# Clustered attention with two mixer layers on one core: batch 1's four one-hot pieces moved back by one tile, their buffer laid under the value copies

## The reference

```python
q_assign = np.argmax(np.einsum('bhsd,hcd->bhsc', q_n, c_n), axis=-1)
k_assign = np.argmax(np.einsum('bhsd,hcd->bhsc', k_n, c_n), axis=-1)
mask = q_assign[:, :, :, None] == k_assign[:, :, None, :]
scores = scale * np.matmul(q, k.transpose(0, 1, 3, 2))
scores = np.where(mask, scores, -1000000000.0)
...
attn = attn / (np.sum(attn, axis=-1, keepdims=True) + 1e-09)
return np.matmul(attn, v).astype(np.float32)
```

## Time and profile before

| | before |
|---|---|
| median of 3 runs | 792.05 us |
| lowest and highest of them | 791.92 and 793.27 us |
| the profiled execution's own time | 792.6 us |
| its span, first to last instruction | 790.7 us |
| mean granted clock of TensorE | 0.996 |
| PE, DVE, ACT, POOL busy | 768.8, 450.1, 361.7, 136.0 us |

### The profile page before, as it was taken

The page is one execution under the profiler, slowest core; times in us unless marked ns, Lnnn a source line. Parts: engine busy times, 40 slices in busy tenths (PEclk is TensorE's granted clock), DMA queues, the critical chain, the costliest instruction groups (busy, mean ns, idle before and its releaser), DMA issues.

```text
span 790.7 us, 12902 instructions
## 1 busy us (share of the span) xinstructions
PE 768.8 (97%) x3997; PEld 659.8 (83%) x3997; DVE 450.1 (57%) x761; ACT 361.7 (46%) x742; POOL 136.0 (17%) x162
## 2 busy tenths in 40 slices
PE   7989999999999889999999999999999999999998
PEld 6878999999999668888888888888888888888886
DVE  4778999999999684333533353334254335334333
ACT  5567888888888533323333233332123233323321
POOL 1351332233228660000300040000300000000000
PEclk9999999999999999999999999999999999999999
DMA  7935354444441223333323323333003333333334
GB/s 246 225 105 134 94 122 103 119 105 119 105 117 33 70 96 101 93 105 83 104 80 106 99 84 110 88 98 106 0 1 107 93 93 94 93 106 84 103 105 173
DMA packets 82840, 81.08 MB, mean 103 GB/s; under 512 B 7296, under 2 KB 69056, under 8 KB 82816
## 3 DMA queue, kind: packets, MB, share of 16 engines
q1 hardware_dynamic: 82816, 80.77, 37.0%
HBM read 56.95 MB, written 4.72 MB: 78 GB/s over the span
## 4 chain that ended last, share of the span: by engine, by line
PE 63%; DVE 2%; ACT 0%; issue 0%
PE bank L998 29%; PE bank L989 29%; PE bank L976 2%; PE bank L957 2%; PE bank L940 1%; DVE kT_hi L1099 1%; DVE x L1117 0%; DVE x L1150 0%; DVE w_lo L1130 0%; DVE uT_lo L1094 0%; DVE w_lo L1089 0%; DVE t L1108 0%; DVE h_lo L1126 0%; ACT qT_hi L1048 0%; ACT h_hi L1067 0%
## 5 line engine op out<-in xcount | busy, mean ns | idle before, releaser
L1126 DVE SCALAR_TENSOR_TENSOR h_lo<-bank,h_hi 128x512 fp32r<-128x512 f32 x84 | 58.1, 692 | 261.8 <-ACT h_hi L1067 261.8
L1067 ACT ACTIVATE h_hi<-bank 128x512 fp32r<-128x512 f32 x84 | 50.2, 598 | 301.4 <-PE bank L989 301.4
L989 PE MATMUL bank<-uT_hi,w_hi 128*128 128x512 f32 x336 | 131.2, 391 | 0.0
L998 PE MATMUL bank<-w_hi,h_hi 128*128 128x512 f32 x336 | 131.1, 390 | 0.0
L989 PE MATMUL bank<-uT_hi,w_lo 128*128 128x512 f32 x336 | 130.8, 389 | 0.0
L989 PE MATMUL bank<-uT_lo,w_hi 128*128 128x512 f32 x336 | 130.8, 389 | 0.0
L998 PE MATMUL bank<-w_hi,h_lo 128*128 128x512 f32 x336 | 130.7, 389 | 0.0
L998 PE MATMUL bank<-w_lo,h_hi 128*128 128x512 f32 x336 | 130.7, 389 | 0.0
L595 DVE TENSOR_TENSOR pT_lo<-back,pT_hi 128x384 fp32r<-128x384 f32 x192 | 98.1, 552 | 6.9 <-ACT pT_hi L496 3.5
L496 ACT ACTIVATE pT_hi<-back 128x384 fp32r<-128x384 f32 x192 | 84.4, 497 | 36.2 <-PE back L740 34.6
L563 DVE TENSOR_REDUCE negmax<-front 128x1 f32<-128x768 f32 x96 | 91.3, 952 | 9.2 <-PE front L639 9.2
(11 more groups left out here) (125 smaller groups left out, 1054.1 us busy)
## 6 DMA issues: line engine op xcount, KB each, us to landing
w_raw<-in_moe_w_ch_dram SPq DMA_DIRECT2D x168, 256.0 KB, 2.9
Q<-qT_hi SPq DMA_DIRECT2D x64, 96.0 KB, 2.2
K<-kT_hi SPq DMA_DIRECT2D x64, 96.0 KB, 2.1
q_raw<-in_q_dram SPq DMA_DIRECT2D x8, 384.0 KB, 6.0
k_raw<-in_k_dram SPq DMA_DIRECT2D x8, 384.0 KB, 7.0
Q<-qT_lo SPq DMA_DIRECT2D x32, 96.0 KB, 2.1
K<-kT_lo SPq DMA_DIRECT2D x32, 96.0 KB, 2.1
v_raw<-in_v_dram SPq DMA_DIRECT2D x16, 192.0 KB, 2.7
```

The source lines that it names most:

```text
L989: last = nc.tensor.matmul(hid[par][:, :], w[par][:, kd, :], y[cc % 2][:, kd, :], start=(kd == 0 and m == 0), stop=(kd == KD - 1 and m == 2))
L998: last = nc.tensor.matmul(acc[k][:, :], y[par][:, k * P:(k + 1) * P], w[par][:, :], start=(start and m == 0), stop=(stop and m == 2))
L1067: nc.scalar.activation(h_hi[par][:, :], hid[par][:, :], ACT.Relu).then_inc(h_hi_made, 1)
L1126: nc.vector.scalar_tensor_tensor(out=h_lo[par][:, :], in0=hid[par][:, :], scalar=0.0, in1=h_hi[par][:, :].bitcast(F32), op0=ALU.max, op1=A ...
```

## The change

The four pieces of batch 1 are done one tile later on both PE and ACT. On PE, pieces 0 to 3 stood behind T 1, S 4, T 2 and S 5; they now stand behind T 2, S 5, T 3 and S 6. On ACT, they stood behind `high` of tile 1, `exp` 3, `high` 2 and `exp` 4; they now stand behind `high` 2, `exp` 4, `high` 3 and `exp` 5. At tile 4 of the first pair, AV part 0 moves from ahead of T 4 to behind it. `onehot1` moves to where `avT` and `av` lie later (a filler named `apart`, never used, sets the distance), since tile 3's exponentials are now written while the buffer is still read. No instruction is added or removed, and DVE, POOL and SP keep their order.

```diff
--- before.py
+++ after.py
@@ -66,6 +66,8 @@
         before, after = {0: ([], []), 1: ([0], [1]), 2: ([2], [])}[part]
         if first and G == 0:
             before, after = [], []
+        elif first and t == GT + 1:
+            before, after = [], [0, 1]
         steps += [("AV", G - 1, p) for p in before] + [("T", t, 0)] + [("AV", G - 1, p) for p in after]
     if last:
         steps += [("F", GPP - 2, 0)] + [("AV", GPP - 1, part) for part in range(AV_PARTS)] + [("F", GPP - 1, 0)]
@@ -138,7 +140,7 @@
 
         with ExitStack() as prep:
             raw = [sb(n, [P, H, NT, D], where=prep) for n in ("q_raw", "k_raw")]
-            onehot = [sb(f"onehot{b}", [P, 2 * NT, H * C], where=prep) for b in range(B)]
+            onehot = [sb("onehot0", [P, 2 * NT, H * C], where=prep)]
             best = sb("best", [P, 2, GROUPS], where=prep)
             first = sb("first", [P, 2, GROUPS], where=prep)
             prio_i = sb("prio_i", [P, C], I32, where=prep)
@@ -148,6 +150,8 @@
             c_n = sb("c_n", [P, 2 * D], where=prep)
             c_st = sb("c_st", [P, 8], where=prep)
             c_blk = sb("c_blk", [P, 2, 2, 4 * (P + C)], F32R, where=prep)
+            sb("apart", [P, GW - 2 * TPP // GT], where=prep)
+            onehot.append(sb("onehot1", [P, 2 * NT, H * C], where=prep))
             simT = [[x[:, i, GW * n:GW * (n + 1)] for n in range(2)] for i in range(2)]
             eq = [x[:, 2 + i, 0:2 * SIMS].rearrange("p (n y) -> p n y", n=2) for i in range(2)]
             ohT = [x[:, 4 + n, 0:S] for n in range(2)]
@@ -506,14 +510,14 @@
                 for t in range(TPP):
                     if t + 1 < TPP or not last_pair:
                         exp(g, t + 1)
-                    if first_pair and t in (2, 3):
-                        onehot_piece(2 * t - 3)
+                    if first_pair and t in (3, 4):
+                        onehot_piece(2 * t - 5)
                     if t % GT == 0 and not (first_pair and t // GT < 2):
                         fin(t // GT - 2)
                     high(t, 0)
                     high(t, 1)
-                    if first_pair and t in (1, 2):
-                        onehot_piece(2 * t - 2)
+                    if first_pair and t in (2, 3):
+                        onehot_piece(2 * t - 4)
                 if last_pair:
                     fin(GPP - 2)
                     fin(GPP - 1)
@@ -724,8 +728,8 @@
                 for kind, n, part in pair_steps(first_pair, last_pair):
                     if kind == "S":
                         scores(g, n)
-                        if first_pair and n in (4, 5):
-                            onehot_piece(2 * n - 7)
+                        if first_pair and n in (5, 6):
+                            onehot_piece(2 * n - 9)
                     elif kind == "T":
                         if first_pair and n == 0:
                             pe.wait_ge(oh_copied, 2)
@@ -740,8 +744,8 @@
                                 last = nc.tensor.transpose(t_bank[i % 3][:, t * P:(t + 1) * P],
                                                            prob[n % 2][:, c:c + P], ident[:, :])
                             last.then_inc(p_tr, 1)
-                        if first_pair and n in (1, 2):
-                            onehot_piece(2 * n - 2)
+                        if first_pair and n in (2, 3):
+                            onehot_piece(2 * n - 4)
                     elif kind == "AV":
 
                         j = n % GPP // 2
```

## The result

The changed kernel took 794.96 us (median of 22 runs), the kernel before 792.54 us (22 runs beside it): ratio 1.0028, interval 1.0018 to 1.0038. It is slower by 2.2 us by the ratio and 2.4 by the medians, beyond rival A's size: the forecast of 793.6 and the range up to 794.6 miss it. That is past the 1.6 us that the prediction set for telling a change; it had given "slower" 0.30 and "same" 0.62. The profiled execution of the changed kernel is the fastest of its 22, 791.32 us (span 789.4).

The account below looks back on a forecast made before the run. PE was taken as full outside its waits, with SP's DMA chain setting pair 1's scores. 792.6 - 0.2 (chain) + 1.5 (low clock) = 793.9, or 793.35 by the median; 793.6 was taken, range 791.7 to 794.6.

Parts of the forecast that it names:

- rival A: The forecast: SP's chain holds and the longer wait at pair 1's scores brings the low clock; 793.35 to 793.9, chance 0.52.
- the stall for POOL is not on the path: At piece 0, PE's 2.58 us wait for POOL goes, but SP's chain to pair 1's scores takes the gain back.
- C: Rival: the wait for POOL at piece 0 is on the path, so removing it gains; 789.6, chance 0.07.
- ACT sets the end of the copies: From 50.8 us ACT does nine jobs, 6.53 us, without waiting; last copy ends at 57.3, against 57.48 before.
- my own sign of being wrong: Wrong if the last copy ends over 0.5 us from 57.3, or pair 1's scores start earlier than SP's chain allows.
- the wait grows to 2.95 and ends at 72.35: At pair 1's scores PE arrives 1.3 us earlier and waits 2.95 us instead of 1.87, until 72.35.
- The low clock comes at the wait: Behind the DMA wait at pair 1's scores the granted clock falls to 0.50 once, for some 3.3 us.
- 15.06 us of one queue, stiff: SP's chain from the last copy to pair 1's scores: fixed at 15.06 us, with nothing hanging on PE.
- -0.2 us (bounds -0.3 and +0.3): SP's chain starts 0.2 us earlier, so pair 1's scores may start at 72.35 instead of 72.54.
- the cost of the low clock: Behind the wait at pair 1's scores, where PE is the bound: +1.5 us, bounds 0 and 1.65.
- the AV move: First AV starts at 57.35 with T 4 behind PE; counted in PE's 1.3 us lead, with no cost of its own.
- Rival D: The new 1.1 us wait in T 2 still brings the low clock at 51 to 55 us; 793.9 or 795.4, chance 0.10.

Follow-up runs that it names:

- e1: The changed kernel with SP issuing the 12 rows of pair 1's first head ahead of the two one-hot stores; 789.14 us, ratio 0.9960.
- c2: The changed kernel, unchanged, run again for another trace; 796.89 us, ratio 1.0054.
- c3: The changed kernel, unchanged, run a third time for one more trace; 793.73 us, ratio 1.0015.
- c4: The changed kernel, unchanged, run once more as partner of the version without the AV move; 795.68 us, ratio 1.0046.
- e9: The changed kernel with AV part 0 left ahead of T 4, as in the kernel before; 791.65 us, ratio 0.9988.
- e9b: A repeat of e9, the changed kernel with AV part 0 left ahead of T 4; 791.49 us, ratio 0.9990.
- e8: The kernel before, old order, with two small unused loads in SP's queue ahead of pair 1's operands; 796.68 us, ratio 1.0038.
- e4: The changed kernel with 8 unread identity transposes ahead of T 2, inside PE's new wait there; 795.82 us, ratio 1.0039.
- e2: The changed kernel with 24 unread identity transposes on PE ahead of pair 1's first scores; 792.19 us, ratio 1.0008.

## Why the prediction was right and wrong

**Right: the stall for POOL is not on the path.** It went, and the time was taken back at pair 1's scores; e1 shows the gain (3 us) once they need not wait. C did not come.

**Right: ACT sets the end of the copies**, with luck in the number. It ran without a gap. The nine jobs took 57.34 - 51.31 = 6.03 us, not 6.53: neighbours overlap by more than the 0.02 each that I took. `exp` 3 started 0.5 later than the 50.8 of the forecast, as T 1 did, and the two errors cancel. By my own sign of being wrong (the last copy more than 0.5 from 57.3) three of the four traces are wrong, at 59.23 (c2), 57.97 (c3) and 59.07 (c4): by where T 1 stands, and c2 by the low clock besides.

**Right in direction, by luck in size: the wait grows to 2.95 and ends at 72.35**, 2.94 and 72.38 in the first trace. There SP's first operand goes out 60.76 - 57.34 = 3.42 us after the last copy, where the kernel before had 2.73, and the operands then take 72.38 - 60.76 = 11.62 to the scores, where it had 12.33: two changes of 0.7 that I had at nothing cancel. **The low clock comes at the wait** in three of four traces. Where it lasts 3.4 us it costs 1.6 and 1.5 us over the first 200 matmuls of pair 1 (term: 1.5, bounds 0 and 1.65).

**Wrong: "From the last copy to the scores are 72.54 - 57.48 = 15.06 us of one queue, stiff: nothing of it hangs on PE."** This is the step that failed, with the term "-0.2 us (bounds -0.3 and +0.3)" made from it. One row gave the length, and I took it for a constant. In the changed kernel's traces it is 15.04, 14.87, 16.30 and 16.36 (mean 15.6), as the last store lands after 3.0, 3.0, 4.3 and 4.4 us; in the other five of the table it is 14.3 to 15.1 (mean 14.6), with the landing at 2.3 in every one. And something of it does hang on PE: e9 and e9b differ from the changed kernel in PE's order alone, and have 14.26 and 14.41. The length, which the sum left unchanged, is up to 1.3 longer than the row it came from, in two traces of four, and this lengthens PE's wait to 4.2.

**Too small: the cost of the low clock.** Its upper bound, 1.65, was half of one stretch of 3.30 us. c4's and e8's lasted 6.8 us and cost 2.3 and 2.9 over the first 200 matmuls of pair 1.

**Wrong by omission: the AV move.** I counted it as part of PE's lead and priced it at nothing. It is the part that loses. With it PE doesn't stand 0.65 us in front of the first AV, so it stands longer at the DMA wait. Without it the wait is 1.5 to 1.7, the store of k's rows lands after 2.3, neither trace has a low clock at the wait, and the kernel takes 791.5 instead of 795. (By their mean clock of 0.995 or 0.996, 9 of e9's and e9b's 23 executions have a second low stretch somewhere.) Of the 1.45 us between the waits of e9 and the changed kernel's first trace, 0.65 are this lead and 0.7 the landing. The expectation of e9, that PE's standing time costs nothing and its lead gains nothing (ratio 1.002 to 1.003), erred in the same way: the lead is worth less than nothing.

**Rival D** (a low clock at T 2) was in one trace of four, and e4 shows that it isn't what makes the median.

By the means of the table the changed kernel is 0.2 behind the three in the old order at the start of pair 1's scores, counted from T 1 (copies 0.7 earlier, chain 0.9 longer), and 1.0 behind in the tail; measured are 2.2 to 2.4. Another 0.8 lies in where T 1 stands (49.7 against 49.0 in these few traces). That looks like chance: over the 18 traces of all kernels T 1 stands at 48.4 to 50.5 in the old order and 48.4 to 50.9 in the new. The tail of the kernel before, 718.2, is 1.1 above its fellows by something between 220 and 317 us, so the old order's own tail may be 717.0. What makes the landing late stays open.

## What to carry to other kernels

A gain ahead of a wait that something else ends is not neutral: it turns into idle time of TensorE at that wait, a longer idle time can bring the low clock, for which the work behind pays, so move the end of that wait first (here SP's queue, ratio 0.996). Measure each hunk of a change by itself: here the pieces alone were at 0.999, with intervals that reach 1.000, and the AV part on top of them lost 3 to 4 us. A latency read from one execution is a sample, not a constant.

## What the runs showed of the hardware

At pair 1's scores the granted clock fell at PE waits of 2.75, 3.10, 4.21, 4.27 and 4.48 us, and not at waits of 1.0 to 2.0 nor at one of 2.94. Elsewhere it fell during the 2.6 us for POOL or up to 1.5 us behind them in every trace of the old order, and once, in c2, behind waits of only 0.71, 0.36 and 1.04 us. So the length of one wait doesn't decide it alone. It stayed at 1.2 GHz for 3.4 us in some executions and 6.8 in others, which cost 1.5 to 1.6 and 2.3 to 2.9 us over the next 200 matmuls. 24 transposes whose result nobody reads, put into the wait, kept the clock at 1.00 there (e2).

The Trainium skill, page "TensorE: Matmul & The Clock Gate", section "HAM oscillation — how this bites in real kernels", prices the low clock at half the throttled time. The stretches give 1.7 and 3.4 by that, so the short ones nearly agree and the long ones cost less; part of each can lie inside the wait, where PE has no work to slow (1.8 us of c4's, 0.5 of e8's).

The same store of 384 KB landed after 2.3 us in six traces and after 3.0 to 4.5 in seven, and in each of the seven one of the sixteen small packets that end it came 0.5 us or more behind the others.
